# A small product inside a two-MLP kernel on quarters of the TensorE array, and 96 bytes behind a buffer

## The reference

```python
# q, k, v: (8 batches, 8 heads, 576 rows, 64)
q_s = softmax(q, axis=-1);  k_s = softmax(k, axis=2)     # over the rows
kv = np.einsum('bhsd,bhse->bhde', k_s, v)                # 64x64 for each head
attn = np.einsum('bhsd,bhde->bhse', q_s, kv)
x = attn.transpose(0, 2, 1, 3).reshape(4608, 512)
h = x @ w_in; g = max(h, 0) + alpha * min(h, 0)          # 512 -> 2048
x = g @ w_out                                            # 2048 -> 512
h = x @ w_in2; s = h * softmax(h); ln = layernorm(s) * g_ln   # 512 -> 1024
out = ln @ w_out2                                        # 1024 -> 512
```

## Time and profile before

| | |
|---|---|
| median of 3 runs | 1295.68 us (1295.67 to 1296.25) |
| the profiled execution | 1295.62 us, of which the trace spans 1293.8 us |
| TensorE busy in the trace | 1281.2 us (99%) |
| first phase (to the last `down`) | about 908 us |
| second phase | about 386 us |

### The profile page before, as it was taken

The page is one execution under the profiler, slowest core; times in us unless marked ns, Lnnn a source line. Parts: engine busy times, 40 slices in busy tenths (PEclk is TensorE's granted clock), DMA queues, the critical chain, the costliest instruction groups (busy, mean ns, idle before and its releaser), DMA issues.

```text
span 1293.8 us, 16928 instructions
## 1 busy us (share of the span) xinstructions
PE 1281.2 (99%) x6277; PEld 1046.4 (81%) x6277; DVE 692.7 (54%) x965; ACT 387.2 (30%) x625; POOL 345.6 (27%) x289
## 2 busy tenths in 40 slices
PE   7999999999999999999999999999999999999998
PEld 6788888888888888888888888888888888888887
DVE  7865744644644644644644323345765555555552
ACT  4333212212222222212212212123544444444432
POOL 5333233233233234134134222223211111111110
PEclk8999999999999999999999999999999999999999
DMA  8543211311311311311310100301554444444432
GB/s 204 139 119 84 83 37 53 90 36 41 101 36 41 102 36 41 102 36 41 102 36 4 66 1 9 122 33 41 186 171 142 143 146 146 146 146 146 146 122 74
DMA packets 136018, 114.82 MB, mean 89 GB/s; under 512 B 56857, under 2 KB 117809, under 8 KB 135089
## 3 DMA queue, kind: packets, MB, share of 16 engines
q1 hardware_dynamic: 135936, 114.37, 30.0%
q10 hardware_dynamic: 48, 0.01, 0.0%
HBM read 76.03 MB, written 38.32 MB: 88 GB/s over the span
## 4 chain that ended last, share of the span: by engine, by line
PE 98%; DVE 1%; DMA 0%; issue 0%; ACT 0%; POOL 0%; DVEq 0%
PE ps_y L1219 10%; PE ps_y L1218 10%; PE ps_h L1201 10%; PE ps_y L1217 10%; PE ps_h L1202 10%; PE ps_h L1203 10%; PE ps_y L1337 5%; PE ps_y L1339 5%; PE ps_y L1338 5%; PE ps_m L1267 3%; PE ps_h L1267 3%; PE ps_m L1268 3%; PE ps_h L1268 3%; PE ps_h L1272 3%; PE ps_m L1272 3%; PE ps_m L1127 2%
## 5 line engine op out<-in xcount | busy, mean ns | idle before, releaser
L527 POOL TENSOR_TENSOR gl<-tg,gh 128x512 fp32r<-128x512 f32 x144 | 192.0, 1333 | 600.2 <-ACT gh L646 600.2
L646 ACT ACTIVATE gh<-tg 128x512 fp32r<-128x512 f32 x144 | 91.1, 633 | 610.5 <-PE ps_y L1219 444.6
L944 DVE TENSOR_SCALAR tg<-ps_h,acols 128x512 f32<-128x512 f32 x144 | 107.7, 748 | 249.9 <-PE ps_h L1203 248.2
L1219 PE MATMUL ps_y<-gh,WO 128*128 128x512 f32 x576 | 228.7, 397 | 0.0
L1217 PE MATMUL ps_y<-gh,WO 128*128 128x512 f32 x576 | 228.3, 396 | 0.0
L1218 PE MATMUL ps_y<-gl,WO 128*128 128x512 f32 x576 | 228.2, 396 | 0.0
L1201 PE MATMUL ps_h<-xh,W 128*128 128x512 f32 x576 | 227.7, 395 | 0.1
L1202 PE MATMUL ps_h<-xl,W 128*128 128x512 f32 x576 | 225.0, 391 | 0.0
L1203 PE MATMUL ps_h<-xh,W 128*128 128x512 f32 x576 | 224.7, 390 | 0.0
L1218 PEld LDWEIGHTS ps_y<-gl,WO 128*128 128x128 f32 x576 | 108.7, 189 | 25.0
L1219 PEld LDWEIGHTS ps_y<-gh,WO 128*128 128x128 f32 x576 | 108.2, 188 | 25.3
(11 more groups left out here) (163 smaller groups left out, 1639.8 us busy)
## 6 DMA issues: line engine op xcount, KB each, us to landing
z_scratch<-zb SPq DMA_DIRECT2D x35, 512.0 KB, 2.6
zt<-z_scratch SPq DMA_DIRECT2D x140, 128.0 KB, 3.0
y_scratch<-stage SPq DMA_DIRECT2D x36, 256.0 KB, 3.1
A<-k_dram SPq DMA_DIRECT2D x16, 512.0 KB, 5.0
V<-v_dram SPq DMA_DIRECT2D x32, 256.0 KB, 4.7
out_dram<-ost SPq DMA_DIRECT2D x32, 256.0 KB, 2.3
A<-q_dram SPq DMA_DIRECT2D x14, 512.0 KB, 5.1
stage<-kx_scratch SPq DMA_DIRECT2D x6, 1024.0 KB, 4.7
```

What stands on the lines that cost most here:

```text
L527: nc.gpsimd.tensor_tensor(gl[:, f % 2, :], tg[:, f % 2, :], gh[:, f % 2, :].bitcast(F32), ALU.subtract).then_inc(gl_ok, 1)
L944: nc.vector.tensor_scalar(tg[:, f % 2, :], ps_h[:, f % 2, :], 0.0, slope[:, f:f + 1], ALU.min, ALU.mult).then_inc(t_ok, 1)
L1219: mm = nc.tensor.matmul(o, WO[:, f, 1, cols], gh[:, f % 2, :], start=False, stop=(f == NF - 1))
```

## The change

1. `x_product` no longer uses `kvh`, `kvl`, `qTh`, `qTl`. It reads the fp32 `kvf` and one fp32 buffer `qT` of four tiles, and does for each pair of k tiles four fp32 matmuls of 64x64 weights by 512 columns. For even j the head from partitions 0 to 63 goes to partitions 0 to 63 and the other to 64 to 127; for odd j the halves are swapped. In the loop even j write `m0` and odd j `m1`. `xr_product` does the same.
2. Because the rows of odd k tiles of x are swapped in halves, each tile of `w_in` is loaded by three transfers instead of one, two of which write the swapped halves.
3. `kv_high`, `kv_low` and `q_low` are gone from ScalarE and VectorE. `xr_copy` is two copies instead of one.
4. The steps on TensorE stand elsewhere: `xr_product` alone at f = 13, `q_transpose` 1 at f = 14, `q_transpose` 2 at f = 15, and the tail is "y", "X0", "y", "y", "T3", "y", "T4", "y", "X1", "y", "y", "y". `x_product` waits for `qh_ok` (the copy of the second tile of its pair) and, from the second on, for `xl_ok` of tile 1; `q_transpose` 3 waits for `xl_ok` of tile 0, since X0 has written `m0`.
5. `pad_v`, 24 floats (96 bytes) per partition, stands behind `V`: what lies behind it up to `acols` starts at a multiple of 128 bytes.
6. TensorE's chunks 1 to 6 are written out instead of looped. `dgh`, `dgl` and the split of x2 have buffers of their own, of the same total size.

```diff
-            qTh = sb("qTh", [P, 2, TOK], F32R)
-            qTl = sb("qTl", [P, 2, TOK], F32R)
+            qT = sb("qT", [P, KT, TOK])
             qR = sb("qR", [P, KT, REM])
             A = sb("A", [P, MAIN + RCOL])
             V = sb("V", [P, TT + 1, H, D + 1])
+            sb("pad_v", [P, 24])
...
-            kvh = sb("kvh", [P, KT, P], F32R)
-            kvl = sb("kvl", [P, KT, P], F32R)
+            dgh = sb("dgh", [P, DM], F32R)
+            dgl = sb("dgl", [P, DM], F32R)
...
-        def x_bank(unit, first):
-            if not first:
-                return m1
-            return ps_y[:, unit - 1, :]
+        def x_bank(j, first):
+            if first:
+                return ps_y[:, j, :]
+            return m0 if j % 2 == 0 else m1
...
+                    dst = stage[:, u % 4, :].rearrange("p (i o n) -> p i o n", i=2, o=2)
+                    src = w_in[:, f * P:(f + 1) * P].rearrange("(i o s d) n -> o s d i n", i=2, o=2, s=2)
+                    sp.dma_start(dst[:, :, 0, :], src[0].rearrange("s d i n -> (s d) i n")).then_inc(w_ld[u % 4], 16)
+                    for s in range(2):
+                        sp.dma_start(dst[(1 - s) * D:(2 - s) * D, :, 1, :], src[1, s]).then_inc(w_ld[u % 4], 16)
...
                     if unit == 1:
-                        pe.wait_ge(qR_ok, b + 1)
+                        pe.wait_ge(xr_ok, b + 1)
+                    elif unit == 3:
+                        pe.wait_ge(xl_ok, 4 * b + 1)
                     else:
-                        pe.wait_ge(ql_ok, 4 * b + unit - 1)
+                        pe.wait_ge(qh_ok, 4 * b + unit - 1)
...
+            def x_product(b, pair, first=False):
+
+                pe.wait_ge(qh_ok, 4 * b + 2 * pair + 2)
+                if pair == 0:
+                    pe.wait_ge(kvf_ok, b + 1)
                     if not first:
                         pe.wait_ge(xr_ok, b + 1)
                 elif not first:
-                    pe.wait_ge(xl_ok, 4 * b + j)
-                hi, lo = q_slot(j, first)
-                nc.tensor.matmul(bank, kvh[:, j, :], hi, start=True, stop=False)
-                nc.tensor.matmul(bank, kvh[:, j, :], lo, start=False, stop=False)
-                nc.tensor.matmul(bank, kvl[:, j, :], hi, start=False, stop=True).then_inc(x_ps, 1)
+                    pe.wait_ge(xl_ok, 4 * b + 2)
+                for j in (2 * pair, 2 * pair + 1):
+                    for lo in (0, D):
+                        to = lo if j % 2 == 0 else D - lo
+                        mm = nc.tensor.matmul(x_bank(j, first)[to:to + D, :], kvf[lo:lo + D, j, :],
+                                              qT[lo:lo + D, j, :], start=True, stop=True)
+                mm.then_inc(x_ps, 1)
...
-                        mm = nc.tensor.matmul(m1[lo:lo + D, j * REM:(j + 1) * REM], kvf[lo:lo + D, j, :],
+                        to = lo if j % 2 == 0 else D - lo
+                        bank = m1 if j % 2 == 0 else m0
+                        mm = nc.tensor.matmul(bank[to:to + D, j * REM:(j + 1) * REM], kvf[lo:lo + D, j, :],
...
-            tail = ["X1", "T3", "y", "y", "X2", "y", "T4", "y", "X3", "y", "y", "y", "X4", "y"]
+            tail = ["y", "X0", "y", "y", "T3", "y", "T4", "y", "X1", "y", "y", "y"]
...
-            with pe.Fori(1, B - 1) as c:
+            for c in range(1, B - 1):
                 chunk(c)
```

More of the change, by code:

```diff
@@ L114, in linear_attention_two_mlps @@
             zt = sb("zt", [P, 2, F2])
+        with ExitStack() as phase:
+            sb("skip_x2", [P, (NF * 2 * KT * P + NF * 2 * DM) + 2 * KT * TOK + KT * REM])
+            x2hb = sb("x2hb", [P, 2, TOK], F32R)
+            x2lb = sb("x2lb", [P, 2, TOK], F32R)
         ps_y = ctx.enter_context(nc.psum_tensor("ps_y", [P, 4, TOK], F32))
@@ L218, in linear_attention_two_mlps @@
               A[:, MAIN:MAIN + DM].rearrange("p (a n) -> p a n", a=KT))
-        x2h, x2l = (t[:, :, :].rearrange("p s (a n) -> p s a n", a=KT) for t in (qTh, qTl))
-        dgh, dgl = qTh[:, 1, :], qTl[:, 1, :]
+        x2h, x2l = (t[:, :, :].rearrange("p s (a n) -> p s a n", a=KT) for t in (x2hb, x2lb))
         kb4 = stage[:, :, :].rearrange("p j n -> p (j n)")
@@ L601, in q_exp @@
                 nc.scalar.activation(flat(Q, piece), flat(Q, piece), ACT.Exp).then_inc(qexp_ok, 1)
[L603 to L610, removed]
             def q_high(b, unit, first=False):
                 act.wait_ge(qt_ps, 5 * b + unit + 1)
-                if not first:
-                    act.wait_ge(x_ps, 4 * b + (unit - 2 if unit >= 3 else 0))
+                if not first and unit > 0:
+                    act.wait_ge(x_ps, 2 * b)
                 bank = q_bank(unit, first)
@@ L621, in q_high @@
                 else:
-                    nc.scalar.activation(q_slot(unit - 1, first)[0], bank, ACT.Copy).then_inc(qh_ok, 1)
+                    nc.scalar.activation(qT[:, unit - 1, :], bank, ACT.Copy).then_inc(qh_ok, 1)
             def xr_copy(b, first=False):
@@ L891, in kv_norm @@
                 if not first:
-                    dve.wait_ge(kvl_ok, b)
+                    dve.wait_ge(x_ps, 2 * b)
                 nc.vector.tensor_tensor(kvf[:, :, :], kv[:, :, 0:D], spread(kr[:, :], D),
                                         ALU.mult).then_inc(kvf_ok, 1)
[L896 to L905, removed]
             def q_max(b, piece, Q, first=False):
@@ L962, in _ @@
             kv_norm(0, first=True)
-            q_low(0, 1, first=True)
-            kv_low(0, first=True)
-            for unit in range(2, KT + 1):
-                q_low(0, unit, first=True)
             for j in range(KT):
@@ L1107, in k_broadcast @@
                 pe.wait_ge(dg_ok, 2 * b + 1)
[L1108 removed]
+                nc.tensor.matmul(m1, ones[:, :], dgh[:, :], start=True, stop=False)
                 pe.wait_ge(dg_ok, 2 * b + 2)
[L1110 removed]
+                nc.tensor.matmul(m1, ones[:, :], dgl[:, :], start=False, stop=True).then_inc(mb_done, 1)
             def kv_product(b, first=False):
@@ L1162, in q_transpose @@
                 mm.then_inc(qt_ps, 1)
-            def x_product(b, unit, first=False):
-                bank = x_bank(unit, first)
-                j = unit - 1
-                pe.wait_ge(ql_ok, 4 * b + unit)
-                if j == 0:
-                    pe.wait_ge(kvl_ok, b + 1)
+            def x_product(b, pair, first=False):
+                pe.wait_ge(qh_ok, 4 * b + 2 * pair + 2)
+                if pair == 0:
+                    pe.wait_ge(kvf_ok, b + 1)
                     if not first:
@@ L1249, in _ @@
                 q_transpose(0, unit, first=True)
-            for unit in range(1, KT + 1):
-                x_product(0, unit, first=True)
+            for pair in range(2):
+                x_product(0, pair, first=True)
             def m1_product(m, r, first=False):
```

63 lines of the change are left out of this document (21 added, 42 removed).

## The result

| | before | after |
|---|---|---|
| median | 1295.68 us (1295.64 to 1296.25, 4 runs) | **1284.07 us** (1283.48 to 1284.88, 4 runs) |
| ratio | | **0.991**, 95% interval 0.9893 to 0.9927 |
| the profiled execution | 1295.62 us, span 1293.8 | 1284.88 us, span 1282.8 |
| start of the first `up` | 28.75 us | 29.17 us |
| chunk 0 | 101.28 us | 100.47 us |

The account below looks back on a forecast made before the run. TensorE, busy 99% of the span, was taken as the bound. 1295.6 - 14.0 (96 bytes) + 1.3 (product and waits, seven blocks) - 0.6 (start) = 1282.3 us; its own range 1279 to 1288, the 8-in-10 range 1279 to 1298.

Parts of the forecast that it names:

- the case: Whole kernel: faster by more than 2.6 us, about 0.2%, the least a measurement can tell from no change; chance 0.62.
- Part 1, the 96 bytes: `down` and the `up` behind it: aligning `gh` and `gl` saves 0.10 us a pair, 144 times, 14.0 us; bounds 0 and 14.4.
- one line of 64 bytes too many: Reads of `gh`, `gl`: a 2048-byte block starting off a 64-byte line touches 33 lines, not 32, costing 0.0067 us a matmul.
- the three supports: Operand places against matmul rates: `gh`/`gl` off and slow, `xh`/`xl` and second-phase operands aligned, `kvh`/`kvl` weights off, `x_product` slow.
- Part 2, the product: Product on TensorE: four quarters at a time, a group costs 1.22 us, `xr_product` 0.23 less; -0.56 us a block in sum.
- Part 3, the waits: TensorE in the tail: new waits for copies and for `xl` cost 0.75 us a block; bounds 0 and 1.5 us.
- 0.30, 0.10, 0.22, 0.13: TensorE's waits in us: X0 for tile 2's copy, T3 for `xl` of tile 0, T4 and X1 for copies of tiles 3 and 4.
- Part 4, the start: Block 0: without `kvl` and `qTl` on the chain X0 starts earlier, -0.6 us; the extra `w_in` transfers count nothing.
- Place not the cause: Rival on `gh` and `gl`: their place does not slow `down`, the 14.0 us stay, 1296.3 us; chance 0.18.
- Two quarters: Rival on the new product: only two quarters run at a time, 15.7 us more over eight blocks, 1298.0 us; chance 0.12.
- One at a time in one bank: Rival on the new product: quarters writing one bank run singly, a group 3.45 us, about 43 us more, 1325 us; chance 0.04.

Follow-up runs that it names:

- experiment 1: The kernel before with only the 96 empty bytes added behind `V`: 1283.06 us, ratio 0.9901.
- experiment 2: The kernel after without the 96 bytes behind `V`: 1296.66 us, ratio 1.0004.
- experiment 5: The kernel before with 32 bytes behind `V`, with 112 there, or with 96 behind `gl` instead: 1296.09, 1297.51 and 1295.91 us, one run each.
- experiment 3: The kernel after with odd k tiles unswapped, so only two diagonal quarters are used, and `w_in` in one transfer a tile: 1298.12 us, ratio 1.0018.
- Experiment 4: The kernel after with `q_transpose` 2 ahead of the `down` of f = 15, its copy ahead of `g_high`, and the tail reordered: 1279.70 us, ratio 0.9874.

## Why the prediction was right, and where not

Predicted 1282.3 us, measured 1284.07: the sign, the case and nearly the size are right; the 1.8 us that are missing lie in two terms.

*Part 1, the 96 bytes: 14.0 forecast, 12.7 measured* (12.8 from experiment 1, 12.6 from experiment 2). That `down` is slow for the place of `gh` and `gl`, and that the `up` behind it pays too, was read rightly from two rates in the trace. Mis-sized is the count: 144 whole pairs at 0.097. An unprepared chunk gains 1.58, a prepared one 1.39 (98.29 - 96.90), since matmuls close behind a transpose or a product on part of the array are as slow with everything in place: the `up` behind `q_transpose` 2 takes 2.85 us in the kernel before and in that of experiment 1. 7 x 1.39 + 2 x 1.58 = 12.9. The reason that I gave, one line of 64 bytes too many, is wrong (experiment 5). Of the three supports, `x_product` bears little: with everything in place its four take 0.69, 0.70, 0.70 and 0.68 us (experiment 1), so that the place of its weights explains at most 0.01 us of the 0.70, and in two of the four nothing.

*Part 2, the product: -0.56 us a block forecast.* The four starts at a time are there (experiment 3 shows what two would be: 1.86 us). A group takes 1.02 from its start to the next line, and with the 0.09 ahead of it (0.32 instead of 0.23) and the slower first matmul behind it (0.34 instead of 0.23) it costs 1.22, as forecast; `xr_product` takes 0.39 us, 0.22 less, where I had 0.23 less. Experiment 4, which has this part without the waits, is 0.46 us a chunk below the 96 bytes alone, against 0.56; of the 0.10 between them 0.04 is that the four old `x_product` take 2.76 us in all in experiment 1, and were priced at 2.80; the rest stays open.

*Part 3, the waits: 0.75 us forecast, 0.64 measured*, and one by one 0.30, 0.10, 0.22, 0.13 against 0.20, 0.11, 0.25, 0.08. Parts 2 and 3 together were to cost 0.19 us a chunk and cost 0.16 (97.06 against 96.90).

*Part 4, the start: -0.6 forecast; +0.8 in the profiled execution, -0.6 in its repeat*, by the start of the second `up` (31.50 before, 32.27 and 30.87 after). From `kv_product` to the second `up` it is 12.71 us in both instead of 13.28, so the step itself gave its 0.6. The step that failed is that I took the start of `kv_product` as fixed at 18.22 us. In six traces of kernels with the new product on four quarters it lay between 18.16 and 19.56; in seven of kernels with the old product it lay between 17.90 and 18.53, and there the first `up` did not follow it. Why it starts later on average with the new code stays open: six traces can't tell chance from cause. The three transfers per `w_in` tile are not it: in experiment 3, with one transfer, the first `up` comes no earlier (29.29 us), and chunk 0 is 3.31 us longer than the chunks behind it, against 3.41 in the kernel after.

*The rivals.* Place not the cause: excluded by experiment 1. Two quarters: it would have been 1298.0 us, and experiment 3, which is that rival made real, took 1298.12. So close a meeting is luck: it lies 14.05 us above the kernel after, where 15.7 were counted, and the 1.8 that the forecast lacks fill the gap. One at a time in one bank: no group of the kernel after came near 2.05 us. In the kernel after, the two quarters that go to different halves of one bank (`m0` for even j) read from different row halves of the array, and four records of a group start within 0.02 us. The Trainium skill, "TensorEngine Tiling (Array Packing)", section "Restrictions and Gotchas", says that different row tiles cannot access one PSUM bank simultaneously; at 512 columns the trace disagrees with it too. Eight records take 1.02 us in all there; on one quarter they follow each other in steps of 0.43 us (experiment 3), which would make 3.44 one by one.

So nearly all of the gain is the empty 96 bytes. The part that looks like the change, the product on quarters, costs about 1 us as it was placed, and brings 3.4 us (1283.06 to 1279.70) once four steps stand elsewhere.

## What to carry to other kernels

When an engine is busy 100% of a stretch, still compare the steps of equal instructions in different places: 0.2342 against 0.2267 us per matmul was worth 12.8 us of 1296, more than everything else in this change. Look at where every operand starts, weights included, and test a gap of a few bytes by itself before counting a rewrite's gain as the rewrite's. A cheaper step on the engine that bounds pays only if what feeds it keeps its cover: write down for each new wait the chain behind it and the work ahead of it, and order the steps by that.

## What the runs showed of the hardware

- In a stream of its own kind, an fp32r matmul of 128x128 weights by 512 columns takes 0.2267 us if both operands start at a multiple of 256 bytes, counted from the start of the first buffer, and 0.233 to 0.234 if one of them, moving or weights, starts at 16, 32, 128, 160 or 192 past one (not every offset was tried for both kinds). Both off cost no more than one. Three to seven matmuls behind slow ones are slow too, which gives an `up` in place 2.73 to 2.76 us; behind a transpose it takes some 2.85, with everything in place too (experiment 1). No run showed the mechanism.
- Four fp32 matmuls of 64x64 weights by 512 columns, one on each quarter of the array and two of them writing halves of the same bank, take 1.02 us together; two on the diagonal at a time make it 1.86.
- In the first 20 us the granted clock of the same kernel at the same moment differed between executions (0.61 and 1.00 from 9 to 10 us), and the first `up` of the one came 1.40 us later than that of the other. Whether the clock alone does it is not shown: the traces of experiments 2 and 4 read 1.00 from 9 to 18 us and start late too. A kernel whose start is bound by VectorE does not show it.
